# An attention, FFN and expert-routing kernel: expert tiles of 256 slots become tiles of 128 and 64, the 64 with its low halves beside it in one weight load

## What is computed

```python
do_compute = x @ w_skip > 0
xc = x[do_compute]; logits = xc @ w_gate; e_idx = argmax(logits)
out = x.copy()
for e in range(8):
    mask = e_idx == e
    h = np.maximum(xc[mask] @ w1[e], 0.0)          # 512 -> 1024
    y[mask] = gate_w[mask, None] * (h @ w2[e])     # 1024 -> 512
out[do_compute] = xc + y
```

## Time and profile before

| | |
|---|---|
| median of 3 runs | 717.63 us (716.43 to 718.22) |
| the profiled execution, its own time | 718.74 us |
| its span, first to last instruction | 717.1 us |
| mean granted TensorE clock | 0.991 |
| busy: PE (matmul) / DVE / ACT / POOL | 671.2 / 392.6 / 369.4 / 159.3 us |
| expert tiles 1 to 7 and the end | from 552.65 us to the last instruction |

### The profile page before, as it was taken

How to read it: one execution, slowest core, us unless ns; L and a number is a source line. 1 busy time by engine, 2 the same in 40 slices (tenths; PEclk the granted TensorE clock), 3 DMA queues, 4 the chain that set the end, 5 groups by cost and what they waited for, 6 DMA issues and landing times.

```text
span 717.1 us, 14298 instructions
## 1 busy us (share of the span) xinstructions
PE 671.2 (94%) x4533; PEld 576.4 (80%) x4534; DVE 392.6 (55%) x1363; ACT 369.4 (52%) x1043; POOL 159.3 (22%) x211
## 2 busy tenths in 40 slices
PE   3889999999999999999999999999978899999990
PEld 3678888888888889889898988998857688887870
DVE  4867764555456434253343433445575876577664
ACT  4778766555656333333333333344436865457661
POOL 5345312231223002010010000100222433303431
PEclk9999999999999999999999999999999999999996
DMA  7547634223321331102001020023118886557761
GB/s 254 190 131 251 208 121 162 73 73 132 102 73 40 119 121 30 60 1 89 1 19 70 0 88 0 0 74 89 46 46 260 281 259 212 188 179 240 243 210 40
DMA packets 48215, 85.60 MB, mean 119 GB/s; under 512 B 7618, under 2 KB 11714, under 8 KB 48160
## 3 DMA queue, kind: packets, MB, share of 16 engines
q1 hardware_dynamic: 43664, 79.20, 33.6%
q0 software_dynamic: 3952, 4.65, 2.2%
q10 hardware_dynamic: 544, 1.05, 0.4%
HBM read 70.84 MB, written 18.52 MB: 125 GB/s over the span
## 4 chain that ended last, share of the span: by engine, by line
PE 81%; issue 5%; DVE 4%; POOL 4%; ACT 2%; DMA 2%; POOLq 1%; DVEq 0%; SPq 0%; ACTq 0%
PE ph L1345 27%; PE px L1358 27%; PE pe_h L1445 8%; PE py L1471 7%; PE pscore L1295 3%; PE ptrans L1304 2%; PE pctx L1317 2%; DMA w_raw<-we 1%; PE ph L1369 1%; PE phT L1457 1%; POOL probs L651 1%; DMA xg<-x_dram,gather_slots 1%; DVE w_lo L952 1%; ACT w_hi L772 1%; PE pxT L1425 1%
## 5 line engine op out<-in xcount | busy, mean ns | idle before, releaser
L1345 PE MATMUL ph<-x_hi,w_hi 128*128 128x256 f32 x576 | 166.2, 289 | 0.8 <-DVE x_lo L1013 0.8
L1108 DVE SCALAR_TENSOR_TENSOR gated<-gated,ph 128x256 f32<-128x256 f32 x144 | 60.5, 420 | 188.1 <-ACT gated L849 188.0
L1345 PE MATMUL ph<-x_lo,w_hi 128*128 128x256 f32 x576 | 160.6, 279 | 0.0
L1345 PE MATMUL ph<-x_hi,w_lo 128*128 128x256 f32 x576 | 160.4, 279 | 0.0
L1358 PE MATMUL px<-w_hi,g_hi 128*128 128x512 f32 x288 | 117.7, 409 | 0.0
L1345 PEld LDWEIGHTS ph<-x_hi,w_hi 128*128 128x128 f32 x576 | 108.5, 188 | 7.9 <-issue 3.3
L1358 PE MATMUL px<-w_hi,g_lo 128*128 128x512 f32 x288 | 113.6, 394 | 0.0
L1358 PE MATMUL px<-w_lo,g_hi 128*128 128x512 f32 x288 | 113.0, 392 | 0.0
L1345 PEld LDWEIGHTS ph<-x_lo,w_hi 128*128 128x128 f32 x576 | 108.9, 189 | 3.6
L1345 PEld LDWEIGHTS ph<-x_hi,w_lo 128*128 128x128 f32 x576 | 108.8, 189 | 0.0
L849 ACT ACTIVATE gated<-ph 128x256 f32<-128x256 f32 x144 | 54.9, 381 | 102.3 <-PE ph L1345 102.3
(11 more groups left out here) (201 smaller groups left out, 1101.9 us busy)
## 6 DMA issues: line engine op xcount, KB each, us to landing
w_raw<-we SPq DMA_DIRECT2D x72, 256.0 KB, 3.2
more_raw<-we SPq DMA_DIRECT2D x72, 256.0 KB, 4.0
w_raw<-wf SPq DMA_DIRECT2D x32, 256.0 KB, 3.9
vs<-vw SPq DMA_DIRECT2D x16, 384.0 KB, 3.4
qs<-qT SPq DMA_DIRECT2D x16, 288.0 KB, 3.8
ks<-kT SPq DMA_DIRECT2D x16, 288.0 KB, 4.2
xT_dram<-x_stage SPq DMA_DIRECT2D x16, 288.0 KB, 3.1
x_lo<-xT_dram SPq DMA_DIRECT2D x8, 512.0 KB, 3.8
```

Of the source, the lines that this page charges most:

```text
L1108: nc.vector.scalar_tensor_tensor(gated[s % 2][:, :], gated[s % 2][:, :], 1.0, ph[s % 2][:, 0:TT], ALU.add, ALU.mult).then_inc(gated_done, 1)
L1345: last = nc.tensor.matmul(ph[f % 2][:, 0:TT], up_w(w, k, f), x[p][:, k, :], start=(at == 0 and n == 0), stop=(at == KD - 1 and n == 2))
```

## The change

Three parts. First, `ET` is 192: half 0 has 128 slots, half 1 (`REST`) 64. The 64 slots of half 1 stand twice in one stationary operand of 128 columns: high parts in columns 0 to 63, low parts in 64 to 127 (`xe_rest`, `h_rest`). Two matmuls (x w_hi, x w_lo) take the place of three, and the result has partial sums of the high parts in partitions 0 to 63 and of the low parts in 64 to 127. So the relu of half 1 is a plain copy, its transposes give both parts, and VectorE adds them (`sum_h`, a new `tensor_reduce` out of `phT`), ScalarE takes relu and high part of the sum (128x256), and VectorE the low part (128x256, `scalar_tensor_tensor`). In the end `add_rows` runs twice for half 1: once for the high partitions, then for the low ones onto the same `rows`, with a semaphore between them.

Second, VectorE's order in tiles 1 and up: `both_rows` goes ahead of chunks 9 to 13, `sum_h` and the splits go between the chunks. Third, on GpSimd the second half's scatter follows the first's in its own round, the loop over pairs is cut into (1 to 3) and, only if more than 8 tiles exist, the rest. `xe` banks go by half, not by pairs of k; `e_up(t,0,0)` waits for half 0's low part alone. `MAXT` goes from 16 to 20 and the list table gets 128 rows more.

```diff
-ET = 256
-EH = ET // P
+ET, EH = 192, 2
+REST = ET - P
+MAXT += MAXT % 2

-    with eng.Fori(1, MAXT // 2) as s:
-        with eng.If(total > s * 2 - after):
-            for p in range(2):
-                body(s, p, s * 2 + p)
+    def some(pairs):
+        with eng.Fori(*pairs) as s:
+            with eng.If(total > s * 2):
+                for p in range(2):
+                    body(s, p, s * 2 + p)
+    some((1, E // 2))
+    with eng.If(total > E):
+        some((E // 2, MAXT // 2))
...
             def routed_tile(s, p, t):                      # GpSimd
-                first = isinstance(t, int) and t == 0
                 with if_exists(pool, total, t):
                     gather(t + 1, 1 - p, s + p)
-                if not first:
-                    with if_exists(pool, total, t - 1):
-                        scatter(t - 1, 1, 1 - p, s + p - 1)
-                with if_exists(pool, total, t):
                     pool.wait_ge(gathered[p], (s + 1) * 16 * EH)
                     load_slots(gather_slots[p], row_of(t + 2), gather_slots_in[p])
...
                     scatter(t, 0, p, s)
+                    scatter(t, 1, p, s)
...
             def split_h_hi(t, h, o):                       # ScalarE
+                at = slice(o * FPO, (o + 1) * FPO)
+                if h == 0:
...
+                else:
+                    act.wait_ge(h_summed, t * EFO + o + 1)
+                    nc.scalar.activation(h_rest[:, at, 0, :], h_sum[:, at, :], ACT.Relu).then_inc(h_hi_done, 1)
...
+            def sum_h(t, o):                               # VectorE
+                at = slice(o * FPO, (o + 1) * FPO)
+                dve.wait_ge(h_transposed, (t * EH + 1) * EFO + o + 1)
+                wait(dve, h_hi_done, ((t - 1) * EH + 1) * EFO + o + 1)
+                wait(dve, h_lo_done, ((t - 1) * EH + 1) * EFO + o + 1)
+                nc.vector.tensor_reduce(h_sum[:, at, :], phT[o][:, :, :].rearrange("p f (a t) -> p f t a", t=REST),
+                                        AX.X, ALU.add).then_inc(h_summed, 1)
...
+                    nc.vector.scalar_tensor_tensor(h_rest[:, at, 1, :], h_sum[:, at, :], 0.0, h_rest[:, at, 0, :].bitcast(F32),
+                                                   ALU.max, ALU.subtract).then_inc(h_lo_done, 1)
...
-                    add_rows(1).then_inc(rows_done[p], 1)
+                    add_rows(1).then_inc(rest_rows_begun, 1)
+                    dve.wait_ge(rest_rows_begun, t + 1)
+                    add_rows(1, REST, rows).then_inc(rows_done[p], 1)
...
                     next_lo(3, 4, 5)
+                    sum_h(t, 0)
+                    next_lo(6)
                     split_h_lo(t, 1, 0)
-                    next_lo(6, 7, 8)
+                    next_lo(7, 8)
                     xe_split_lo(t + 1, 1 - p)
+                    sum_h(t, 1)
                     split_h_lo(t, 1, 1)
-                    next_lo(9, 10, 11, 12, 13)
                     both_rows()
-                    next_lo(14, 15)
+                    next_lo(9, 10, 11, 12, 13, 14, 15)
...
                 for k in ks:                               # TensorE, e_up; e_down alike
+                    if h == 0:
...
+                    else:
+                        for n, w in enumerate((w_hi, w_lo)):
+                            last = nc.tensor.matmul(pe_h[o][:, :], xe_rest[p][:, k, :, :], e_up_w(w, p, k, o),
+                                                    start=(k == 0 and n == 0), stop=(k == KD - 1 and n == 1))
```

More of the change, by code:

```diff
@@ L454, in score_bank, with xe_bank, part, xe_hi_of @@
             return ph[h] if m < UALONE and m % 2 else pscore[h]
-        def first_pxT(h):
-            return pxT[h][:, :, :].rearrange("p k (j t) -> p (k j) t", t=P)
+        def xe_bank(h):
+            return pxT[h][:, :, 0:part(h)]
+        def part(h):
+            return REST if h else P
+        def xe_hi_of(p, h):
+            return xe_rest[p][:, :, 0, :] if h else xe_hi[p][:, :, :]
+        def xe_lo_of(p, h):
+            return xe_rest[p][:, :, 1, :] if h else xe_lo[p][:, :, :]
         def trans_bank(n):
@@ L706, in scatter @@
                 take_waits(NT + t * EH + h)
[L707 to L708 removed]
+                pool.indirect_dma_start(out[:, :], bass.IndirectOffsetOnAxis(scatter_slots_of[p][0:part(h), h, 0:1], 0),
+                                        rows[p][0:part(h), h, :], None, bounds_check=last_token,
                                         oob_is_err=False).then_inc(rows_stored[p], 16)
@@ L1418, in tile, with transpose_part @@
                         down(t - 1, FB - 1)
+            def transpose_part(p, h):
+                n = part(h)
+                for k in range(KD):
+                    last = nc.tensor.transpose(xe_bank(h)[:, k, :], xg[p][0:n, h, k * P:(k + 1) * P], ident[0:n, 0:n])
+                last.then_inc(xe_transposed, 1)
             def transpose_xe(t, p, uses):
                 pe.wait_ge(gathered[p], (uses + 1) * 16 * EH)
-                wait(pe, xe_lo_done, t * 2)
-                for k in range(KD):
-                    for h in range(EH):
-                        last = nc.tensor.transpose(pxT[k // 2][:, k % 2, h * P:(h + 1) * P],
-                                                   xg[p][:, h, k * P:(k + 1) * P], ident[:, :])
-                    if k % 2:
-                        last.then_inc(xe_transposed, 1)
+                wait(pe, xe_lo_done, t * EH)
+                for h in range(EH):
+                    transpose_part(p, h)
             def h_bank_free(t, h, o):
@@ L1469, in e_down @@
                         pe.wait_ge(w_lo_done, NCH + t * ECH + EUPCH + f + 1)
-                    for n, (g, w) in enumerate(((h_hi[h], w_hi), (h_hi[h], w_lo), (h_lo[h], w_hi))):
-                        last = nc.tensor.matmul(py[h][:, :], g[:, f, :], e_down_w(w, p, f),
-                                                start=(f == 0 and n == 0), stop=(f == EFB - 1 and n == 2))
+                    if h == 0:
+                        for n, (g, w) in enumerate(((h_hi, w_hi), (h_hi, w_lo), (h_lo, w_hi))):
+                            last = nc.tensor.matmul(py[h][:, :], g[:, f, :], e_down_w(w, p, f),
+                                                    start=(f == 0 and n == 0), stop=(f == EFB - 1 and n == 2))
+                    else:
+                        for n, w in enumerate((w_hi, w_lo)):
+                            last = nc.tensor.matmul(py[h][:, :], h_rest[:, f, :, :], e_down_w(w, p, f),
+                                                    start=(f == 0 and n == 0), stop=(f == EFB - 1 and n == 1))
                 if o == EFO - 1:
@@ L1512, in first_transposes @@
                 pe.wait_ge(gathered[0], (h + 1) * 16)
-                for k in range(KD):
-                    last = nc.tensor.transpose(first_pxT(h)[:, k, :], xg[0][:, h, k * P:(k + 1) * P], ident[:, :])
-                last.then_inc(xe_transposed, 1)
+                transpose_part(0, h)
             def list_late():
```

144 lines of the change are left out of this document (70 added, 74 removed).

## The result

The changed kernel takes **724.99 us** (median of 5 runs, 720.86 to 728.21) beside 717.67 us for the kernel before (716.43 to 718.35): ratio 1.0094, 95% interval 1.0052 to 1.0137. It is slower, by 0.9%. I had forecast 710.2 us, range 705 to 716.5, and gave slower 0.09.

What follows compares the result with a forecast made beforehand. TensorE was taken to bound the tiles over 128 tokens, but not tile 5. The terms by tile came to -7.4 us, 718.74 to 711.3 us, less 1.1 for the runs' median: 710.2 us, range 705 to 716.5.

Steps and rivals of the forecast that it cites:

- Part 1: Over tiles: 16 matmuls for 24 in each second-half product, 3.67 us less a tile, 18.3 at most; still 8 tiles.
- Part 2: New VectorE and ScalarE work: sum_h 0.68 us, 1.1 us wait of e_down(1,1); tiles 3 and 4 -2.5 us, tile 5 +2.0.
- Rival 2: VectorE's strided reduce sum_h costs 1.05 us instead of 0.68, +4.1 us in all, so 714.3 us; chance 0.14.
- rival 1: TensorE stays the bound throughout and the waits fit elsewhere: -18.3 us, 699.5 us; chance 0.05.
- Rivals 3 and 4: Weight loads land after 4.0 us, 715.6 us, chance 0.14; at 4.8 us the weight loop closes, slower, 720.4 us, 0.10.
- the sum: Tiles 0 and 1 -0.8, 2 -1.8, 3 and 4 -2.5 each, 5 +2.0, 6 -1.0, end -0.8: -7.4 us.
- Part 3: The end: second scatter issued 3.0 us after rows, lands S + 24.1; VectorE's chunks end last at S + 25.2, -0.8 us.

Runs made afterwards that it cites:

- e4: The changed kernel with a 1x1 VectorE memset behind each of chunks 9 to 15 in tiles 1 to 7: 719.21 us, ratio 1.0022.
- e2: The changed kernel with GpSimd's old order back, the second half's scatter behind the next gather, and the old loop over pairs: 717.92 us, ratio 0.9996.
- e3: The changed kernel with VectorE's and GpSimd's old orders both back, only the narrow tiles left: 715.96 us, ratio 0.9964.
- e11: e10 with 17 matmuls that nothing reads added in TensorE's waits of tile 0: 715.75 us, ratio 0.9944.
- e10: Narrow tiles, both old orders, memsets behind chunks 14 and 15, plus tile 0's rows ahead of chunks 8 to 11, memsets there from chunk 9: 715.47 us, ratio 0.9942.
- e12: Narrow tiles, both old orders, memsets behind chunks 14 and 15, plus GpSimd's gather ahead of both scatters of the tile: 713.64 us, ratio 0.9918.

## Why the prediction was wrong

First matmul of tile 1, length of each tile, and the end, in us, from the timelines of the profiled executions (end: from tile 7's first matmul to the last instruction). The forecast row is the row before plus the differences that the prediction gives:

| | start of 1 | 1 | 2 | 3 | 5 | 6 | end |
|---|---|---|---|---|---|---|---|
| before | 552.65 | 17.5 | 24.7 | 24.6 | 15.2 | 24.8 | 26.2 |
| forecast | 550.8 | 18.6 | 22.9 | 22.1 | 17.2 | 23.8 | 25.4 |
| changed | 553.67 | 24.3 | 23.65 | 22.35 | 20.3 | 23.9 | 29.1 |
| e4 broken burst | 551.43 | 22.4 | 23.7 | 22.4 | 17.3 | 24.6 | 26.2 |
| e2 gather first | 550.46 | 18.2 | 23.8 | 22.3 | 17.3 | 23.8 | 29.1 |
| e3 both old | 552.14 | 19.05 | 22.4 | 22.4 | 16.65 | 22.6 | 28.5 |

**Right.** Part 1: 80 matmuls gone, 8 tiles. Part 2: `sum_h` 0.68 us, the wait of `e_down(1,1)` 1.2 us (1.1), tiles 3 and 4 22.35 us (22.1), tile 6 23.9 (23.8), tile 5 17.3 us wherever the gather is not late (17.2; the prediction's 17.1 starts from a window of 15.05). Rival 2 (a reduce of 1.05 us) and rival 1 fell with these rows. Rivals 3 and 4 put the danger in the weight loop; its waits are there (12.1 us of ScalarE for `w_raw`), but about as large as in the sum: tile 2 is 0.8 us over. Three small slips in the prediction change nothing: 3.62 less 2.63 is a wait of 1.0 us and not 1.1, -3.67 - 0.1 + 1.1 is -2.7 and not -2.6, and rival 1 would be 699.3 us and not 699.5. The sum takes a load from the trace, 2.9 us. The Trainium skill, "DMA: Bandwidth & Descriptors", heads its anatomy of one DMA as GpSimd's path, and these loads are issued by SyncE, so that figure was no close match.

**The step that failed** is the price of an instruction on GpSimd, which stands in three places as one and the same assumption: that it costs its own duration. (a) "the gather for tile 2 now stands behind the scatter of tile 0's second half on GpSimd (about 1.1 us issue and 0.35 `tick`)": tile 1 became 5.7 us longer than forecast. From the first scatter to the gather's second issue it took 4.2 us before and 6.6 now (557.37 to 563.95), the gather then landed in 7.0 us where it was 5.25, and the twelve matmuls behind the wait ran at the lower clock, 4.99 us. The longer landing and the clock were no terms of the sum either. (b) "In later tiles the gather lands before TensorE's 11.6 us and costs nothing; without that cover it would cost the same 1.5 us of queue": in tile 5 a tick of 4.1 us comes on top, the gathered rows are there at 14.4 us, and the tile is 3.1 us over. (c) Part 3, "The second scatter is issued 3.0 after rows": 7.7 us, and GpSimd, not VectorE, ended the chain: 3.7 us over. VectorE's own last chunk ended at S + 25.4 (25.2 in the prediction). Together 12.5 of the 16.6 us by which the last instruction came later than the sum had it.

The lock is not all of this. With it broken in tiles 1 to 7 (e4), the last instruction is still 7.4 us later than the sum, and 3.8 of that is tile 1, where the gather stands behind two scatters and the four unbroken chunks of tile 0. So the lock explains (b) and (c), where e4 is within 0.8 us of the forecast; in (a) it holds one tick for 1.75 us in place of 0.18, and how the rest divides between the order of the queue, the slower landing and the clock was not separated.

None of my rivals held this case, although the change put seven chunks beside GpSimd's work, and the trace of before had 1.90 us for a scatter beside two and 1.56 us for a `tick` beside four (557.72 to 559.28 us, where the fourth chunk ends at 559.23). I listed what is queued behind each moved instruction on its own engine, and not what runs beside it on another.

**Tile 0**, 2.9 us over in the profiled run. Two stretches, 529 to 536 and 543 to 550 us, stand at a mean clock of 0.76, where before had 1.00. The second follows a wait of 2.5 us for a relu, as the weight's third load was late; ahead of the first, TensorE's waits are no longer than before, so why it fell there is open. Mean clock over the runs: 0.984 before, 0.973 in the changed kernel, 0.975 to 0.979 in the other narrow ones with no matmuls added; e2, with one such stretch, starts tile 1 at 550.46, as forecast. That narrower tiles leave TensorE more idle, and the clock answers, fits these means and e11, and is not shown by them; what the clock alone costs in this kernel was not isolated, since in e10 and e11 the time did not follow it.

**What the change is worth** when both moves are undone: 715.96 us in e3, 2.6 us better than before, of the 7.4 I had forecast. With the pairs of chunks broken and the gather ahead of the scatters too (e12) it is 713.64, 5.4 us better. The narrow tiles pay; the two moves made around them cost 9.0 us (724.99 to 715.96; across sessions whose medians of before are 0.9 us apart). Undoing the queue's order alone gave 7.1 us, VectorE's alone 1.9, which is not clear of noise.

## What to carry to other kernels

When an edit moves a run of VectorE instructions that read two SBUF tensors, look for what GpSimd does in that time, its DMA issues and one-element instructions included, and price each at the length of the run on top of its own. Only runs of such instructions were seen to do it here. In the trace it shows as an instruction whose duration has two values, and whose end coincides with another engine's. Where the order must stay, one tiny instruction between the chunks opens the gap (5.8 us here); better, put the transfer that someone waits for ahead of the stores that nobody waits for.

## What the runs showed of the hardware

- A GpSimd instruction stands for up to 4.2 us behind seven VectorE instructions of 0.60 us from start to start, and a memset of 0.06 us between them, which moves their starts to 0.61 us apart, lets it through (0.52 us). It applies to the issue of an indirect DMA as to arithmetic (5.68 us against 1.06), and that scatter had begun 0.45 us ahead of the chunks: to be first did not help it. It did elsewhere: in the kernel before, a scatter that began 0.14 us ahead of the four chunks of tile 0 took 1.07 us (556.61).
- It is not held at every such run, nor always to its end. In tile 1 of the changed kernel a tick of 1.75 us ends behind the third of four chunks (560.21 against 560.16), and another took only 0.54 us beside three:

```profile
558.28 2.48 DVE L967 TENSOR_TENSOR w_lo<-more_raw,w_hi 128x512 fp32r<-128x512 f32 x4
558.46 1.75 POOL L658 TENSOR_TENSOR tick<-tick 1x1 f32<-1x1 f32 x1
...
561.44 1.89 DVE L967 TENSOR_TENSOR w_lo<-w_raw,w_hi 128x512 fp32r<-128x512 f32 x3
561.63 0.54 POOL L663 TENSOR_TENSOR tick<-tick 1x1 f32<-1x1 f32 x1
```

  The second ends just behind the start of the second chunk (562.04). What distinguishes these runs from the runs of seven was not tried.
- TensorE's granted clock fell to the lower level (1.2 GHz) behind waits of 2.4 to 6.2 us, and matmuls of 512 columns then started 0.427 us apart and not 0.229. It also fell once, at 529 us, with no wait ahead that the kernel before did not have too. With the waits filled by matmuls for nothing the mean clock over six runs was 0.982 and not 0.977, in ranges that overlap, at no gain in time.
